# Reordering a mixture-of-experts kernel: a weight's low part between table steps, transposes and counts moved, matmul blocks from narrow to wide

## The reference

```python
# retention, causal: B, H, S, D = 4, 8, 768, 64
state = gamma * state + k_t v_t^T ;  y_t = scale * q_t state
x = y as (3072, 512)
# mixture of experts, top 1 of 8: D, F = 512, 1024
logits = x @ w_gate + modality_bias[modality_id]
e = argmax(logits) ;  gate = softmax(logits)[e]
x = gate * (relu(x @ w1[e]) @ w2[e])
# bilinear layer
out = ((x @ wa) * (x @ wb)) @ w3 @ w_out
```

## Time and profile before

| | |
|---|---|
| runs | 906.17, 908.06, 908.53 us; median 908.06 |
| the profiled execution | 903.79 us, of which the span is 902.1 us |
| PE busy | 863.2 us (96%), mean granted clock 0.991 |
| DVE, ACT, POOL busy | 286.5, 258.8, 85.1 us |
| retention (about) | 0 to 115 us |
| wc and the token order | 115 to 174 us |
| expert windows | 174 to 500 us |
| bilinear layer | 500 to 902 us |

### The profile page before, as it was taken

The page is one execution under the profiler, slowest core; times in us unless marked ns, Lnnn a source line. Parts: engine busy times, 40 slices in busy tenths (PEclk is TensorE's granted clock), DMA queues, the critical chain, the costliest instruction groups (busy, mean ns, idle before and its releaser), DMA issues.

```text
span 902.1 us, 13555 instructions
## 1 busy us (share of the span) xinstructions
PE 863.2 (96%) x5236; PEld 740.8 (82%) x5237; DVE 286.5 (32%) x495; ACT 258.8 (29%) x460; POOL 85.1 (9%) x106
## 2 busy tenths in 40 slices
PE   5999999898979999999998999999999999999995
PEld 5888778787979998888888788888888888888884
DVE  2566679540302234121237231121221230230210
ACT  2445523331212243121236322222222221231210
POOL 1222002202020220202000001001001001001001
PEclk9999999999999999999999999999999999999998
DMA  9999751422030243111136102002002002001000
GB/s 331 362 340 367 283 210 47 141 94 95 1 95 0 93 145 134 47 46 47 46 139 187 47 1 80 14 1 82 12 0 81 12 0 93 0 0 47 1 13 35
DMA packets 44008, 85.01 MB, mean 94 GB/s; under 512 B 7744, under 2 KB 8256, under 8 KB 43968
## 3 DMA queue, kind: packets, MB, share of 16 engines
q1 hardware_dynamic: 33376, 60.33, 18.9%
q0 software_dynamic: 4736, 14.72, 5.1%
q10 hardware_dynamic: 5856, 9.40, 3.0%
HBM read 63.42 MB, written 21.00 MB: 94 GB/s over the span
## 4 chain that ended last, share of the span: by engine, by line
PE 89%; DVE 5%; issue 2%; DMA 1%; ACT 1%; ACTq 1%; POOL 0%; DVEq 0%
PE bank L382 77%; PE pair L754 3%; PE bank L771 3%; PE bank L744 2%; PE pair L832 1%; DMA mbias<-n_moe_modality_bias_dram 1%; PE bank L762 1%; PE bank L783 1%; DVE w3T L953 1%; ACT xTu L553 0%; DVE in_lane L1088 0%; DVE wc L1022 0%; DVE we_p L953 0%; ACTq L337 0%; DVE prob L971 0%
## 5 line engine op out<-in xcount | busy, mean ns | idle before, releaser
L382 PE MATMUL bank<-yT,wab 128*128 128x512 f32 x1152 | 262.2, 389 | 1.7 <-issue 1.7
L382 PEld LDWEIGHTS bank<-yT,wab 128*128 128x128 f32 x1152 | 216.1, 188 | 46.7 <-issue 1.9
L382 PE MATMUL bank<-xT,we_p 128*128 128x512 f32 (+2 forms) x768 | 154.2, 361 | 11.3 <-issue 7.5
L382 PEld LDWEIGHTS bank<-xT,we_p 128*128 128x128 f32 x768 | 136.8, 192 | 28.4 <-issue 10.0
L382 PE MATMUL bank<-hT,we_p 128*128 128x512 f32 (+2 forms) x768 | 153.6, 357 | 0.0
L382 PEld LDWEIGHTS bank<-hT,we_p 128*128 128x128 f32 x768 | 132.8, 188 | 14.6
L382 PE MATMUL bank<-wc,gT 128*128 128x512 f32 x576 | 131.5, 389 | 0.0
L382 PEld LDWEIGHTS bank<-wc,gT 128*128 128x128 f32 x576 | 108.1, 188 | 22.5
L1229 DVE TENSOR_TENSOR g<-bank,acopy 128x512 f32<-128x512 f32 x48 | 33.2, 692 | 258.8 <-PE bank L382 258.8
L1190 DVE SCALAR_TENSOR_TENSOR hT<-bank,hT 128x512 fp32r<-128x512 f32 x64 | 44.1, 691 | 171.1 <-ACT hT L632 167.9
L632 ACT ACTIVATE hT<-bank 128x512 fp32r<-128x512 f32 x64 | 38.2, 598 | 113.6 <-PE bank L382 110.3
(11 more groups left out here) (144 smaller groups left out, 544.8 us busy)
## 6 DMA issues: line engine op xcount, KB each, us to landing
we_raw<-in_moe_w_dram SPq DMA_DIRECT2D x6, 2048.0 KB, 9.2
yT_sorted<-yout ACTq DMA_DIRECT2D x8, 1024.0 KB, 4.4
qkv<-in_q_t_dram SPq DMA_DIRECT2D x24, 256.0 KB, 3.8
qkv<-in_v_dram SPq DMA_DIRECT2D x24, 256.0 KB, 5.4
x_rows<-x_keep SPq DMA_DIRECT2D x24, 256.0 KB, 5.3
ytile<-yT_sorted SPq DMA_DIRECT2D x6, 1024.0 KB, 5.0
qkv<-in_k_t_dram SPq DMA_DIRECT2D x23, 256.0 KB, 5.3
qkv<-in_k_dram SPq DMA_DIRECT2D x20, 256.0 KB, 5.7
```

Of the source, the lines that this page charges most:

```text
L382: i = pe.matmul(out_, left(a), right(b), start=(first and n == 0), stop=(last and n == 2), **kw)
```

## The change

It moves work and changes no operation. `counts` goes from step 6 of product 0 to step 0 of product 1. `first_x` goes from step 6 of product 7 to step 2. On DVE `wc_lo(4)` and `w3_lo(6)` go from behind `s_tab` to a place amid the table, after L1141. Chunk 1 of `w1_lo(0)` follows chunk 0 directly. The three copies of the window's code stand in the order 2, 3, 4.

```diff
-            w3_product(0, {2: lambda: rows_and_logits(NT - 1, False), KF - 2: counts})
+            w3_product(0, {2: lambda: rows_and_logits(NT - 1, False)})
...
                 size = table(pe, w, SIZE, 1, GT)
-                with pe.If(size > 3):
-                    wide(4)
-                with pe.If(size < 4):
-                    with pe.If(size > 2):
+                with pe.If(size < 3):
+                    wide(2)
+                with pe.If(size > 2):
+                    with pe.If(size < 4):
                         wide(3)
-                    with pe.If(size < 3):
-                        wide(2)
+                    with pe.If(size > 3):
+                        wide(4)
...
             for f in range(1, KF):
-                w3_product(f, {KF - 2: first_x} if f == KF - 1 else {})
+                w3_product(f, {1: {0: counts}, KF - 1: {2: first_x}}.get(f, {}))
...
             link(dve.tensor_reduce(w_k[:, 0, :], finish, AX.X, ALU.add))
+            wc_lo(4)
+            w3_lo(6)
             link(tt(tmp, start, per_e(TBASE), ALU.add))
...
             w1_lo(0, early_chunks(3))
-            for f in range(4, KF):
+            w1_lo(0, early_chunks(4))
+            for f in range(5, KF):
                 if f == KF - 1:
                     x_lo(0, range(KD))
                 wc_lo(f)
```

## The result

| | before | changed |
|---|---|---|
| median of 11 runs | 906.85 us (904.62 to 909.79) | 903.01 us (901.17 to 905.75) |
| profiled execution, its span | 903.79, 902.1 us | 903.01, 901.3 us |
| mean granted clock | 0.991 | 0.989 |

The ratio of the runs is 0.9955, 95% interval 0.9941 to 0.9969. That is 4.1 us less (3.8 between the medians), and the interval just clears the 0.3% that counts as no change. The two profiled executions differ by 0.8 us only. Why is a question for the experiments.

A forecast was written before the change was run, and what follows sets the result against it. PE, busy 96% of the span, bounds the kernel, so only its stands and slow clock can be won. Terms -2.8 - 10.6 + 9.4 + 1.6 + 0.5 = -1.9 us give 906.2 us, own range 903.5 to 909.8, with rivals 900.3 to 910.5.

The forecast's parts named there:

- Case B: Window 0: two branches wait for code, 3.4 to 6.5 us each, total change -4.6 to +1.7 us; chance 0.50.
- Counts and the low part of w3: wc stage: PE's waits for counts and w3_lo(6) go, product 7 waits 0.9 us; both edits together -2.8 us.
- x(0) sooner: End of wc stage: earlier transposes bring nothing by themselves; the 0.93 us before the first window stays.
- The gain of the blocks: Windows 1 and 2: stands of 2.33 and 5.18 us go and the clock does not fall (3.1 us); -10.6 us.
- The price: Window 0: two taken branches over unused blocks each wait 4.71 us for code, +9.4 us.
- The clock behind it: Window 0: after the long stand the clock falls once, +1.6 us.
- Small: Windows 2, 3, 4 and the exit: extra branches at window starts cost +0.5 us together.
- A: Window 0: only one branch misses, total -6.6 or -7.9 us, result 900 to 901.5 us; chance 0.25.
- C: Loop returns at windows 4, 5, 6: code does not stay, +11 us, 919 us; chance 0.10.
- C2: All seven loop returns: every taken branch waits, +30 us on the forecast, 936 us; chance 0.02.
- D: wc stage: the front gain does not come, as w3_lo(7) and w1_lo are pushed later; up to 2.8 us lost; chance 0.08.
- E: Window 0: misses of over 7 us under the full load, total +2.7 us and more; chance 0.05.

The follow-up runs named there:

- table_only: The kernel before with only DVE's order changed: wc(4) and w3(6) amid the table, w1 chunk 1 behind chunk 0; wc stage 55.72 us in one profile, 1.73 less.

## Why the prediction was right and where it was off

The predicted 906.2 us lies 3.2 above the measured 903.01, inside the range. Case B, the likeliest, was what happened, two branches that wait, though one took 7.0 us where B had 6.5 at most. The size of the change was not met: the forecast was -1.9 us, with "same" the likeliest at 0.42, and 4.1 were measured. Of the 3.2 us, 1.2 are the base, since the three runs shown had a median of 908.06 and the eleven one of 906.85. The mean stages above give -1.9 us too, but that is in part luck, since the terms below miss in both directions; and the 2 us between the stages and the runs stay open.

- *Counts and the low part of w3.* Forecast -2.8 us. Measured 57.45 to 54.97, -2.5, with 0.2 us in front of product 3 and 0.91 in front of product 7 (0.9 forecast). Product 3 ended at 140.29 instead of 140.05 us, and product 7 with its transposes took 7.46 us instead of 7.2. (The steps as written, 140.05 + 5.27 + 11.0, make 156.3 and not the 156.5 named for the end of product 5; products 4 and 5 took 11.2 us before, which gives 156.5.) What I missed is that counts alone could cost time, 2.8 us in the one profile of it, since I priced stands in the wc stage without the clock.
- *x(0) sooner.* Forecast nothing; measured nothing.
- *The gain of the blocks.* Forecast -10.6 us, taken from one execution. Here the sum was mis-sized: in the five other profiles with the old order the two stands are 3.4 to 3.9 and 5.1 to 5.7 us, and the stretch is 1.9 us longer in their mean. I took the first profile for the typical one, though it lay under all three runs shown. With the mean of all six in place of the first, the 10.6 us would be 12.2.
- *The price.* Two branches at window 0 as forecast, 4.71 each: measured 7.0 and 3.34, 10.3 in all against 9.4. The first met the 2 MB load and the gather, the second hardly did. The sequencer came 0.9 us sooner, so window 0 began at 180.34 (180.5 forecast), and the stand grew from 0.93 to 9.79 us, by 8.9.
- *The clock behind it.* Forecast +1.6, measured 29.97 - 27.49 = 2.5.
- *Small.* Forecast +0.5; measured 0.23 us at window 3, 0.44 at window 4, 0.3 at the exit: 1.0.
- *Rivals.* A (one miss) is out by the two branches. C and C2 are out: from 212 to 500 us no packet came on the queue q8, and the later branches took 0.2 us. The rule of the Trainium skill (Runtime: NRT & Kernel Launch, Instruction fetch mechanics), that a taken branch outside two pages waits for its fetch, fits here only the first visits and the one long branch out of `wide(3)` in the old order. D is out by the wc stage. E came for one branch (7.0 us) but not for two.

## What to carry to other kernels

Code is data that has to arrive: lay out the copies of a branched loop so that the first pass runs straight on and each later target lies behind what ran last, and keep bulk loads away from a jump into new code. Judge a stand in front of TensorE by what it leaves behind: in one profile here a wait longer by 0.6 us came with half the clock for microseconds, so an edit that only lets the engine arrive sooner may lose. And compare stages, over more than one profile, before trusting a term that was read from one execution.

## What was not expected

A stand and a slow clock do not go together one to one. In the wc stage 2.72 us left the clock at 1.00 and 3.35 us brought it to 0.50. In front of window 1 it fell after 2.33 us in the first profile of before, and in `table_only` it stayed at 1.00 after 3.47 us:

```profile
216.20 3.47 issue
219.66 21.09 PE bank L382 x120
```

The loss behind a stand was 0 to 2.8 us in these profiles. So the length of a stand alone did not decide it; what did is not shown.
